# Five steps moved on the scalar and vector queues of a fused attention, token mixer and Fourier mixer kernel

## What is computed

```python
def reference(q, k, v, lam, ...):
    out = _attn_ref(q, k, v, lam)            # per head: decayed linear attention in blocks of 64
    x = out as (B, S, 512)
    xt = x.transpose(0, 2, 1)                # token mixer
    u = x + (relu(xt @ w_tok1) @ w_tok2).transpose(0, 2, 1)
    x = u + relu(u @ w_ch1) @ w_ch2          # channel MLP, 512 -> 1536 -> 512
    mixed = real(fft(fft(x, axis=1), axis=2))
    u = x + mixed
    un = (u - mean(u)) / sqrt(var(u) + 1e-6) # over the last axis
    return u + relu(un @ w_ch1b) @ w_ch2b    # channel MLP, 512 -> 2048 -> 512
```

## Time and profile before

| | us |
|---|---|
| median of 3 executions (580.04 to 580.83) | 580.37 |
| the profiled execution, whole | 580.83 |
| its span, first to last instruction | 579.0 |
| PE busy | 565.3 |
| DVE busy | 359.7 |
| ACT busy | 253.2 |
| POOL busy | 244.6 |

### The profile page before, as it was taken

The page is one execution under the profiler, slowest core; times in us unless marked ns, Lnnn a source line. Parts: engine busy times, 40 slices in busy tenths (PEclk is TensorE's granted clock), DMA queues, the critical chain, the costliest instruction groups (busy, mean ns, idle before and its releaser), DMA issues.

```text
span 579.0 us, 9534 instructions
## 1 busy us (share of the span) xinstructions
PE 565.3 (98%) x3602; PEld 501.1 (87%) x3602; DVE 359.7 (62%) x634; ACT 253.2 (44%) x510; POOL 244.6 (42%) x241
## 2 busy tenths in 40 slices
PE   7999999999999999999989999999999999999997
PEld 6889887989898987899869978998888988989996
DVE  5676868676643895376969953769754643443333
ACT  2565434655544453334454533344453344344330
POOL 3342236366634453304767533047654333333311
PEclk9999999999999999999999999999999999999999
DMA  8980211422322120211112202111212122221142
GB/s 306 378 309 3 72 37 42 141 66 72 92 74 72 56 73 19 73 55 55 37 56 72 74 19 73 56 54 37 74 54 91 55 74 72 74 64 50 52 145 110
DMA packets 24157, 49.11 MB, mean 85 GB/s; under 512 B 2472, under 2 KB 3632, under 8 KB 24112
## 3 DMA queue, kind: packets, MB, share of 16 engines
q1 hardware_dynamic: 23520, 46.70, 23.8%
q0 software_dynamic: 448, 1.71, 1.0%
q10 hardware_dynamic: 144, 0.10, 0.1%
HBM read 45.35 MB, written 3.15 MB: 84 GB/s over the span
## 4 chain that ended last, share of the span: by engine, by line
PE 77%; DVE 16%; issue 3%; ACT 2%; DMA 1%; SPq 0%; DVEq 0%; ACTq 0%
PE banks L1095 12%; PE banks L1094 12%; PE banks L1093 12%; PE banks L1358 10%; PE banks L1360 9%; PE banks L1361 9%; DVE al L705 3%; PE banks L1172 2%; PE banks L1118 2%; PE banks L1181 2%; DVE u L875 2%; PE banks L1154 2%; DVE snap L992 1%; DVE h0l L778 1%; PE banks L1197 1%
## 5 line engine op out<-in xcount | busy, mean ns | idle before, releaser
L338 POOL TENSOR_TENSOR w2l<-raw,w2h 128x512 fp32r<-128x512 f32 x56 | 75.6, 1350 | 160.6 <-ACT w2h L453 160.6
L1358 PE MATMUL banks<-th,al 128*128 128x384 f32 x392 | 132.5, 338 | 1.2 <-DVE snap L992 0.4
L1360 PE MATMUL banks<-tl,ah 128*128 128x384 f32 x392 | 132.2, 337 | 0.0
L1361 PE MATMUL banks<-th,ah 128*128 128x384 f32 x392 | 132.0, 337 | 0.0
L453 ACT ACTIVATE snap<-banks 128x384 f32<-128x384 f32 x84 | 41.2, 491 | 137.0 <-PE banks L1361 129.8
L705 DVE TENSOR_TENSOR al<-raw,ah 128x512 fp32r<-128x512 f32 (+1 forms) x112 | 89.6, 820 | 5.0 <-ACT ah L453 3.9
L992 DVE TENSOR_TENSOR snap<-banks,snap 128x384 f32<-128x384 f32 x84 | 46.4, 552 | 65.9 <-PE banks L1361 65.5
L1358 PEld LDWEIGHTS banks<-th,al 128*128 128x128 f32 x392 | 73.6, 188 | 11.2 <-issue 3.1
L1360 PEld LDWEIGHTS banks<-tl,ah 128*128 128x128 f32 x392 | 73.5, 188 | 5.9
L1361 PEld LDWEIGHTS banks<-th,ah 128*128 128x128 f32 x392 | 73.6, 188 | 0.0
L338 POOL TENSOR_TENSOR raw<-raw 128x256 f32<-128x256 f32 x84 | 69.9, 848 | 2.2
(11 more groups left out here) (172 smaller groups left out, 890.6 us busy)
## 6 DMA issues: line engine op xcount, KB each, us to landing
raw<-w1b_dram SPq DMA_DIRECT2D x16, 512.0 KB, 3.2
raw<-w2b_dram SPq DMA_DIRECT2D x32, 256.0 KB, 3.0
raw<-w1a_dram SPq DMA_DIRECT2D x12, 512.0 KB, 3.2
raw<-w2a_dram SPq DMA_DIRECT2D x24, 256.0 KB, 3.2
kTs<-kT_dram SPq DMA_DIRECT2D x8, 384.0 KB, 6.0
qTs<-qT_dram SPq DMA_DIRECT2D x8, 384.0 KB, 7.0
kns<-kn_dram SPq DMA_DIRECT2D x8, 384.0 KB, 7.5
vns<-vn_dram SPq DMA_DIRECT2D x8, 384.0 KB, 5.4
```

Source lines behind the costliest of these rows:

```text
L338: return nc.gpsimd.tensor_tensor(o, i0, i1, ALU.subtract)
L1358: mm(o[:, 0:HALF], al[:, a, cols], th[b][:, t, k, :], start=start and k == 0, stop=False, skip_group_check=True)
L1360: mm(o[:, 0:HALF], ah[:, a, cols], tl[b][:, t, k, :], start=False, stop=False, skip_group_check=True)
L1361: last = mm(o[:, 0:HALF], ah[:, a, cols], th[b][:, t, k, :], start=False, stop=(k == 1), skip_group_check=True)
```

## The change

It moves steps within the ACT and the DVE queue. No instruction is added or taken away, and the queues of PE, POOL and SP hold the same instructions in the same order.

1. ACT: the copy `t1h` stands after head 5 instead of after head 3.
2. ACT, ch 1 and 2: `fold_hi` of the third fold stands at the end of j = 1, ahead of `snapshot(p, 0)` of j = 2, instead of behind it; `side_hi(ch, 2, 0)`, the high part of the first `dft1`, stands behind `up_first_hi` instead of ahead of it.
3. DVE, ch 1 and 2: `fold_lo` of the third fold stands at the end of j = 1, ahead of the first hidden sum of j = 2, instead of behind it.
4. DVE, j = 4 and 5: the second hidden sum stands behind the first `ln_norm` of the pair instead of ahead.
5. DVE, ch 1 alone, j = 5: `up_second_lo` stands ahead of the parts of units 4 and 5 instead of behind them.

```diff
--- before.py
+++ after.py
@@ -481,7 +481,7 @@
                     turned = bank[k][:, at:at + (s1 - s0) * L].rearrange("p (s b d) -> p s b d", b=B, d=D)
                     copy(xh[:, :, cols].rearrange("p (b s) d -> p s b d", b=B)[:, s0:s1, :, :], turned)
                     copy(u[:, :, cols].rearrange("p (b s) d -> p s b d", b=B)[:, s0:s1, :, :], turned).then_inc(u_placed, 1)
-                if h == 3:
+                if h == H - 3:
                     act.wait_ge(s_tokw, 32)
                     copy(t1h[:, :, :], t1raw[:, :, :]).then_inc(tok1h, 1)
             copy(t2h[:, :, :], t2raw[:, :, :]).then_inc(tok2h, 1)
@@ -634,8 +634,6 @@
                 ch, j = place(p)
                 fourier = ch in (1, 2)
                 snapshot(p, 0)
-                if fourier and j == 2:
-                    fold_hi(ch - 1, 2)
                 if p >= 2:
                     down_hi(p - 1, 1)
                 snapshot(p, 1)
@@ -643,15 +641,12 @@
                 if p:
                     act.wait_ge(down_done, 12 * (p - 1) + 3)
                 relu_hi(h0h[:, first], snap[:, 0, :])
-                if fourier and j == 2:
-                    side_hi(ch, j, 0)
                 up_first_hi(p + 1)
                 if ch == 0 and 1 <= j <= 4:
                     n = j - 1
                     act.wait_ge(s_craw, 16 * (n + 1))
                     copy(consts[n][1][:, :, 0:consts[n][4]], cview(n)).then_inc(ch_ready, 1)
-                if not (fourier and j == 2):
-                    side_hi(ch, j, 0)
+                side_hi(ch, j, 0)
                 side_hi(ch, j, 1)
                 snapshot(p, 2)
                 if fourier and j == 1:
@@ -681,6 +676,7 @@
                     edge_row(ch - 1)
                 if fourier and j == 1:
                     row_hi(ch - 1)
+                    fold_hi(ch - 1, 2)
                 side_hi(ch, j, 4)
                 side_hi(ch, j, 5)
                 if units[5] and units[5][0] == "b2":
@@ -1003,7 +999,6 @@
                 if fourier and j == 1:
                     fold_even(ch - 1, 1)
                 if fourier and j == 2:
-                    fold_lo(ch - 1, 2)
                     hidden_lo(p - 1, 4, h0l[:, second], snap[:, 1, :], h0h[:, second])
                 if fourier and j == 3:
                     side_lo(ch, j, 0)
@@ -1025,12 +1020,12 @@
                 if not (fourier and j in (2, 3)):
                     side_lo(ch, j, 0)
                 side_lo(ch, j, 1)
-                if not (fourier and j == 1):
-                    hidden_sum(p, 2, 2, 5)
                 if fourier and j == 4:
                     ln_norm(ch - 1, 0)
                 if fourier and j == 5:
                     ln_norm(ch - 1, 1)
+                if not (fourier and j == 1):
+                    hidden_sum(p, 2, 2, 5)
                 if p == 0:
                     token_out(1, 4)
                     token_out(1, 5)
@@ -1060,8 +1055,7 @@
                     fold_even(ch - 1, 2)
                     fold_lo(ch - 1, 1)
                     fold_odd(ch - 1, 2)
-                ahead = (fourier and j == 3) or (ch == 1 and j == 5)
-                if ahead:
+                if fourier and j == 3:
                     side_lo(ch, j, 4)
                     side_lo(ch, j, 5)
                 up_second_lo(p + 1)
@@ -1070,9 +1064,10 @@
                         add_out(ch - 1, t)
                 if fourier and j == 1:
                     row_lo(ch - 1)
+                    fold_lo(ch - 1, 2)
                 if fourier and j == 4:
                     ln_stats(ch - 1, 1)
-                if not ahead:
+                if not (fourier and j == 3):
                     side_lo(ch, j, 4)
                     side_lo(ch, j, 5)
             for t in range(NC - 1):
```

## The result

| | before | changed |
|---|---|---|
| median, us | 580.21 | 588.33 |
| lowest and highest | 580.04 to 580.83 | 587.9 to 589.1 |
| profiled execution, whole | 580.83 | 587.73 |
| its span | 579.0 | 585.9 |

The ratio is 1.0139 with a 95% interval of 1.0121 to 1.0157: slower by 8.1 us. The forecast was 586.6 with a range of 583.6 to 588.0, so the direction was right, and the time lies 0.3 us above the range. That margin is smaller than the 1.4 us by which the executions of the changed kernel differ: three of the five (587.73, 587.9 and 587.91) lie inside the range. What follows asks which term of the sum was too small.

The account below looks back on a forecast made before the run. PE was taken to bound the kernel, so only its waits and clock could change. Terms 3.4 + 1.0 - 0.7 + 0.9 + 1.6 = +6.2 us on 580.83 gave 587.0, lowered by 0.46 to 586.6 us; range 583.6 to 588.0.

Parts of the forecast that it names:

- What bounds the kernel: Whole kernel: PE's work plus 13.7 us in which PE stands; the change can only shorten or lengthen PE's waits.
- Edit 1, +3.4: Token mixer: the later `t1h` copy delays POOL's `t1l`, so PE's first matmul on it starts 3.4 us later.
- The clock, +1.6: Behind the pause at `t1l`: PE's idleness drops the clock to half rate for a while, costing 1.6 us.
- Rival (a): Behind the pause at `t1l`: the clock doesn't fall, so the time is 585.0 us; chance 0.33.
- Edits 2 and 3, +1.0: Both `dft1` of j = 2, ch 1 and 2: POOL holds the `e` pair, `tph` comes later; +0.5 us each channel.
- Edit 4, -0.7: j = 5, ch 1 and 2: S4's delay is covered, `al` gets ahead of POOL, unit 3 starts earlier; -0.35 us each.
- Edit 5, +0.9: End of ch 1: `up_second_lo` makes units 4 and 5 1.2 us late, some regained at S2; +0.9 us.
- The sum: Whole kernel: 3.4 + 1.0 - 0.7 + 0.9 + 1.6 = +6.2 us, forecast 586.6 us.
- Rival (b): Folds and `up_second_lo`: POOL holds neither, 3.1 us less; 583.5 us with the clock's fall, 581.9 without; chance 0.12.
- Rival (c): Dearest ends of the bounds, with `tpl` and the transposes both later: about 588.0 us; chance 0.06.
- The signs: Expected trace: PE idle 3.3 us before `t1l`, 0.35 then 0.15 more at `dft1`, S4 waiting 0.9, ch 2 about 1.2 late.
- The range: Whole kernel: 583.6 to 588.0 us, said to leave out the cheaper alternatives and the tip of the dearest.

Follow-up runs that it names:

- edit 1 alone: Kernel before with only ACT's copy `t1h` moved behind head 5: 586.04 us, ratio 1.0091.
- edit 5 alone: Kernel before with only DVE's `up_second_lo` moved ahead of units 4 and 5 in ch 1, j = 5: 582.42 us, ratio 1.0042.
- the two held starts: Kernel before with only `up_second_lo` moved, plus POOL's two `w2l` in ch 2's first pair waiting for DVE: 581.74 us, ratio 1.0014.
- the third fold, moved and held together: Kernel before with third fold early, `side_hi` still ahead of `up_first_hi`, POOL held until DVE finished the `e` pair: 578.56 us, ratio 0.9966.
- the run with 12 added matmuls: Changed kernel with 12 identity matmuls on PE ahead of its wait for `t1l`: 587.16 us, ratio 1.0113.

## Why the time lies above the range, step by step

- **What bounds the kernel**: right. All that changed shows in PE's waits and in its clock.
- **Edit 1, +3.4**: right. PE stands 3.40 us, released by POOL's `t1l`. It starts at 52.50 and not at 53.5 because attention ran 1.06 us earlier than in the profiled execution before. `qdec` behind `t1l` cost nothing.
- **The clock, +1.6**: right in the changed kernel's profiled execution, but by luck. The term was built on the length of the warm-up, and the granted clock reads 1.00 from 0 to 12 us of that trace, so its row says nothing of a low clock. It was no bound either: the low stretch is 3.4 us in some executions and 6.8 in others, and the second costs 1.5 more. The prediction's upper end for the stretch, the warm-up's 4.28, was too short. Rival (a), that the clock holds, occurred in no execution of the changed kernel or of edit 1 alone, all at 0.994 to 0.997; of the five of the changed kernel without edit 5, one read 1.000, and it was the shortest, 584.55.
- **Edits 2 and 3, +1.0**: the mechanism is right at both places, the pair held twice and `tph` behind `ah`. (The row of the first `dft1` names no releaser, only "issue"; that the pair on `e` ends the wait was inferred, and the trace of edit 5 alone names it.) The size was 0.8. The wait of S2 for `snapshot(p, 0)`, put at "nothing, or 0.1", was that in ch 1; in ch 2 it was 0.75, through edit 5's lag.
- **Edit 4, -0.7**: the sign is right, the size was 0.4. The shorter `al` freed 0.6 on DVE, but unit 3 was only 0.2 behind PE's own pace, so the 0.35 could not be had.
- **Edit 5, +0.9**: this is the step that failed. Its part that I worked out was 0.85. What I left out is that DVE leaves ch 1 late in respect of POOL, and that two later starts in j = 0 of ch 2, which DVE had won by 0.23 and 0.37 us, are lost by it. I had said "1.2 late, and all of unit 5 behind it" and then counted only until PE's next layer. The term is 2.4 us, in three parts: 0.85 by S2 of j = 0 in ch 2, 0.60 in j = 1 and 0.99 at S2 of j = 2. Three runs show it: edit 5 alone, its absence from the changed kernel, and the two held starts, which take 1.6 away.
- **The sum**: in the two traces, leaving out the 1.06 of attention, the steps give 8.0 us, where the prediction has 6.2. Edit 5 makes 1.5 of the 1.8, edit 4 0.3, the folds take 0.2 back, and 0.2 are the rest of the pause. With the median before, 580.21 + 8.0 = 588.2, and 588.33 was measured.
- **Rival (b)** was wrong for the kernel as it is and right as a statement of what the lock costs: as soon as POOL was held, the folds gained.
- **Rival (c)** comes nearest by its number, about 588.0, but not by its mechanism: it has `tpl` and the transposes later, and the transposes were not.
- **The signs**: all those of "What would show it" came about as to place. They end with the first products of ch 2, so none could catch this miss.
- **The range**: its upper end came from the bounds of single edits, all of them priced where the edit stands. None of them held a cost that arises 10 to 40 us later. At its lower end it leaves out both values of rival (b), 583.5 and 581.9, and not only the lower half.

## What to carry to other kernels

When a step makes an engine late, follow that engine, not only the one that waits for it, until its lag against the others is gone; look on the way for operations that two engines start within a few tenths of a microsecond of each other. Where a DVE operation with two inputs in SBUF starts within 0.4 us of POOL's `w2l`, which of them starts first decided about 1 us each time here, and a wait on POOL for the end of DVE's operation bought that back: 1.6 us for two places, and 0.88 a layer for the third fold, moved and held together. POOL, busy for 42% of the span, had the time to spare. A wait that vanishes from one place counts as a gain only when the next thing that PE asks for is ready earlier too.

## What the runs showed of the hardware

- Which of two operations starts first decides how long the DVE one takes. The text above the prediction calls semaphores the only tie between the queues; these rows show a second one, between DVE and POOL. `h0l` of 128x384 took 0.68 us when it started 0.23 ahead of POOL's `w2l` and 1.65 when `w2l` started 0.07 ahead; the `al` of 128x256 took 0.41 and 1.53 in the same way. The Trainium skill, "SBUF — State Buffer", section "Who interferes with whom", calls this a lock held for a whole instruction, and these rows agree: both held operations ended 0.3 to 0.4 behind the end of POOL's.
- Behind the same pause of 3.40 us the granted clock was at 1.2 GHz for 3.4 us in one execution and for 6.8 in another, and in the run with 12 added matmuls it fell at 340.2 us, in the second of two waits of 0.73 and 1.08 us, for 3.4 us, although the changed kernel's profiled execution has waits of 0.75 and 1.08 there and keeps 1.00. What decides between these cases was not settled.
- The attention stage differs from execution to execution, at pauses of PE for which the profile names no releaser; the cause is not shown: in the changed kernel without edit 5 the same product stood 1.85 us later at 41 us than in the changed kernel, whose attention is the same. Two profiled executions differ by that before an edit has done anything, so terms are best read as differences between places, not from the start of the span.
